# A three-layer kernel: up steps split around the first half of the down step, y's rest copied whole, and another order of roundings, splits and turnings

## The chip, the cores and the metric

The kernel runs on one core of a Trainium2 chip. The metric is device time in microseconds, the median of three runs. Five engines work side by side: PE (matrix products, with PEld for its weight loads), DVE and ACT (elementwise work out of both memories), POOL (elementwise work in SBUF) and SP (which issues all DMAs here).

## The reference

A causal convolution of 7 taps per head (softmax weights) is followed by two dense blocks, each with an up product to 2048 columns, a gate, and a down product back to 192.

```python
w = softmax(weight, axis=-1)                          # [8 heads, 7 taps]
x = conv(x_pad, w)                                    # [8192 tokens, 192]
h = x @ moe_w_in                                      # up 1, to 2048
g = where(h >= 1, h, where(h <= -1, 0, (h + 1)**2 / 4))
y = g @ moe_w_out                                     # down 1, back to 192
h = y @ moe2_w_in                                     # up 2
out = (h * sigmoid(1.702 * h)) @ moe2_w_out           # down 2
```

Everything is fp32. The kernel splits each factor of a product into a rounded part (hi) and its residue (lo) and adds three products of these.

## The kernel before, in words

**Tiles and steps.** The 8192 tokens are 16 tiles of 512. A step is one tile and one of 16 column blocks of 128 (F_TILES); `Step.n` counts steps from 0 to 255. Block 1 works on step n while block 2 works on step n - 24 (BEHIND). The time between two steps is called a slot here, and s is its number within a tile. Slots 0 to 23 are solo slots with block 1 alone. From slot 24 on, slots are paired. Tiles 0 to 3 are written out (`run_head`), tiles 4 to 13 are a loop of pairs, the rest is `run_tail`.

**A paired slot on PE.** Each product is cut into two halves of 64 rows of the array. One block works in the lower half while the other works in the upper half, then they change sides, which is called the flip here. A slot issues `end_up` of the step before (10 products, from L743), `begin_up` (8, from L717), then `down_both` for the step two slots back (LAG): a first half of 10 (L775 to L801), the flip, and a second half of 10 (L805 to L817). That is 38 products of half height, or 19 pairs. Behind a flip, PE waits for its own earlier products into the same bank: L805 waits `main_half` (set by L791), L807 `main2_half` (L793), L813 `rest_half` (L800), L815 `rest2_half` (L801), L743 `h1_half` (L731).

**What feeds it.** In each slot ACT runs two gelu passes of block 2 (L998, L1001), the square (L984) and the rounding of the gate (L990, g_hi). DVE runs the residue of the gate of the step before (L1153, g_lo), the clip (L1138), block 2's residue (L1159) and the gate (L1147). The first down product with g_lo is L791.

**The border of a tile.** When tile t's last down step has ended, ACT copies y's main part (L1008) and the upper half of the rest (L1010, into `y_part`); DVE takes the main residue (L1169), adds the lower half of the rest out of PSUM (L1173) and later takes the rest's residue (L1177); ACT rounds the rest (L1013). The next tile's down step starts in the same banks: L775 waits for L1169, L796 for L1173. That is slot s = 2.

**x of the next tiles.** POOL convolves (`convolve`, L532 and L539), SP moves blocks through DMAs (`move_x`), DVE turns them (`turn_x`, L1197), ACT rounds (`round_x`, L1035) and DVE splits (`split_x`, L1203, L1206), in slots named by the tables EARLY (tiles from 3), MIDDLE (tile 2) and LATE (tile 1).

**The start.** x of tile 0 is turned on PE out of two loads, the main part and the halo (`x_halo`), and convolved on DVE, ACT and POOL. Weights come in 16 chunks: ACT rounds chunk n (`split_weights`, L1044, in the slots of SPLIT_SLOTS), then POOL takes its residue (L564, L565, L568, L587), or DVE for chunk 0 (L1222). POOL also convolves tile 1, helped by ACT (SECOND_SLOTS); PE turns that tile in slot FIRST_PREP_STEP = 15 (`transpose_x`, L910), and step 16 needs it.

## Time and profile before

| what | value |
|---|---|
| runs (3) | 1156.56 us median, 1155.65 to 1156.84 |
| profiled execution | 1157.11 us, span 1155.4 us |
| PE busy | 1138.2 us (99%) |
| DVE, ACT, POOL busy | 822.9 (71%), 699.5 (61%), 446.7 (39%) us |
| mean granted TensorE clock | 0.999 |
| solo slots 0 to 23 | about 16 to 82 us |
| paired slots 24 to 255 | 82 to 1086 us |
| tail, block 2 alone | 1086 to 1155 us |

Matmuls are pipelined, so a product's length (0.39 us) is not its cost; the distance between starts is. The profile's busy share of PE therefore says little, and the time has to be read from distances between starts in the timeline.

### The profile page before, as it was taken

The page shows a single profiled execution, that of the slowest core. Times are in us where ns is not written, and L with a number is a line of the kernel's source. Part 1 is how long each engine was busy: PE and PEld are TensorE (multiplying, and loading weights), DVE is VectorE, ACT ScalarE, POOL GpSimd, SP SyncE. Part 2 cuts the span into 40 slices and gives each one's busy share as a digit, 9 for nine tenths or more (in the row PEclk, how much of TensorE's full clock was granted, in tenths as well). Part 3 has the DMA queues.
Part 4 walks back from the last instruction along what each step waited for, and adds up shares of the span by engine and source line. Part 5 has one row for each costly group of instructions (what it writes and reads, how often), then busy time and mean ns, then how long its engine had stood idle before and what let it go on. Part 6 is the DMA issues. An engine that isn't in the chain of part 4 may idle for free.

```text
span 1155.4 us, 25586 instructions
## 1 busy us (share of the span) xinstructions
PE 1138.2 (99%) x9384; PEld 1024.1 (89%) x9384; DVE 822.9 (71%) x1191; ACT 699.5 (61%) x1213; POOL 446.7 (39%) x441
## 2 busy tenths in 40 slices
PE   7999999999999999999999999999999999999998
PEld 4767899999989999899999999989999999989987
DVE  6877777777777777776777777777777777766633
ACT  5876566566666566565566666565665565655554
POOL 5997654170723608054170622608044180000000
PEclk9999999999999999999999999999999999999999
DMA  6312102020020200102020020200202010000000
GB/s 196 99 37 76 42 12 57 3 53 12 11 53 1 57 7 15 49 4 58 3 51 13 10 54 2 56 8 15 49 3 58 3 17 14 10 6 1 15 7 23
DMA packets 108790, 36.43 MB, mean 32 GB/s; under 512 B 101012, under 2 KB 105490, under 8 KB 108688
## 3 DMA queue, kind: packets, MB, share of 16 engines
q1 hardware_dynamic: 108688, 34.93, 12.7%
q8 instruction: 81, 1.33, 0.5%
q14 instruction: 21, 0.17, 0.0%
HBM read 23.09 MB, written 6.29 MB: 25 GB/s over the span
## 4 chain that ended last, share of the span: by engine, by line
PE 89%; POOL 4%; DVE 2%; SPq 1%; ACT 1%; DMA 1%; issue 1%; DVEq 0%; POOLq 0%; ACTq 0%
PE acc_all L810 4%; PE acc_all L805 4%; PE acc_all L813 4%; PE h_all L743 4%; PE acc_all L808 4%; PE acc_all L816 4%; PE h_all L748 4%; PE h_all L750 4%; PE acc_all L793 4%; PE h_all L746 4%; PE h_all L752 4%; PE acc_all L787 4%; PE acc_all L789 4%; PE h_all L726 4%; PE h_all L728 4%; PE h_all L733 4%
## 5 line engine op out<-in xcount | busy, mean ns | idle before, releaser
L998 ACT ACTIVATE g_hi<-h_all 128x512 fp32r<-128x512 f32 x256 | 153.1, 598 | 203.1 <-PE h_all L754 177.5
L1159 DVE TENSOR_TENSOR g_lo<-h_all,g_hi 128x512 fp32r<-128x512 f32 x256 | 176.7, 690 | 121.2 <-ACT h_all L1001 120.2
L1153 DVE TENSOR_TENSOR g_lo<-gate,g_hi 128x512 fp32r<-128x512 f32 x232 | 184.4, 795 | 110.2 <-ACT g_hi L990 104.3
L990 ACT ACTIVATE g_hi<-gate 128x512 fp32r<-128x512 f32 x232 | 146.5, 631 | 169.3 <-DVE gate L1147 166.0
L1138 DVE TENSOR_SCALAR clip<-h_all 128x512 f32<-128x512 f32 x256 | 175.9, 687 | 51.4 <-PE h_all L752 47.3
L532 POOL TENSOR_TENSOR x_conv<-x_in,tap_w 128x384 f32<-128x384 f32 (+1 forms) x29 | 30.1, 1058 | 458.2 <-DVE x_rest_a L1206 238.0
L539 POOL TENSOR_TENSOR x_conv<-x_conv,prod 128x384 f32<-128x384 f32 (+1 forms) x174 | 203.8, 1192 | 1.6
L984 ACT ACTIVATE clip<-clip,half 128x512 f32<-128x512 f32 x256 | 183.0, 715 | 17.6 <-DVE clip L1138 16.7
L1147 DVE TENSOR_TENSOR gate<-h_all,clip 128x512 f32<-128x512 f32 x232 | 160.4, 691 | 13.2 <-ACT clip L984 7.3
L1001 ACT ACTIVATE h_all<-h_all 128x512 f32<-128x512 f32 x256 | 151.8, 593 | 0.0
L532 POOL TENSOR_TENSOR prod<-x_in,tap_w 128x384 f32<-128x384 f32 (+1 forms) x174 | 149.8, 884 | 3.2
L546 POOL TENSOR_TENSOR raw<-raw,y_part 64x512 f32<-64x512 f32 x15 | 19.3, 1287 | 189.9 <-ACT y_part L1024 189.9
L807 PE MATMUL acc_all<-g_hi,w_down 64*128 64x512 f32 x231 | 91.0, 394 | 0.0
L799 PE MATMUL acc_all<-g_hi,w_down 64*128 64x512 f32 x231 | 90.7, 393 | 0.0
L805 PE MATMUL acc_all<-g_hi,w_down 64*128 64x512 f32 x231 | 90.6, 392 | 0.0
L796 PE MATMUL acc_all<-g_hi,w_down 64*128 64x512 f32 x231 | 90.4, 392 | 0.1
L800 PE MATMUL acc_all<-g_lo,w_down 64*128 64x512 f32 x231 | 90.5, 392 | 0.0
L811 PE MATMUL acc_all<-g_lo,w_down 64*128 64x512 f32 x231 | 90.5, 392 | 0.0
L791 PE MATMUL acc_all<-g_lo,w_down 64*128 64x512 f32 x231 | 89.8, 389 | 0.7 <-DVE g_lo L1153 0.4
L813 PE MATMUL acc_all<-g_hi,w_down 64*128 64x512 f32 x231 | 90.1, 390 | 0.0
L815 PE MATMUL acc_all<-g_hi,w_down 64*128 64x512 f32 x231 | 90.1, 390 | 0.0
L808 PE MATMUL acc_all<-g_hi,w_down 64*128 64x512 f32 x231 | 90.0, 390 | 0.0
(282 smaller groups left out, 4757.6 us busy)
## 6 DMA issues: line engine op xcount, KB each, us to landing
x_in<-in_x SPq DMA_DIRECT2D x14, 960.0 KB, 4.8
out_y<-raw SPq DMA_DIRECT2D x360, 16.0 KB, 1.4
raw<-x_conv SPq DMA_DIRECT2D x336, 16.0 KB, 1.8
raw<-in_moe_w_out SPq DMA_DIRECT2D x6, 384.0 KB, 3.6
raw<-in_moe_w_in SPq DMA_DIRECT2D x4, 512.0 KB, 4.4
raw<-in_moe_w_in SPq DMA_DIRECT2D x8, 256.0 KB, 4.6
stage<-in_moe_w_out SPq DMA_DIRECT2D x2, 384.0 KB, 6.9
x_in<-in_x SPq DMA_DIRECT2D x1, 768.0 KB, 9.0
```

Source lines behind the costliest of these rows:

```text
L532: ins = nc.gpsimd.tensor_tensor(by_head(dst, j), by_head(x_in, k + j), w, ALU.mult)
L539: ins = nc.gpsimd.tensor_tensor(o, o, prod[k % 2][:, j:j + slabs, 0:width], ALU.add)
L805: nc.tensor.matmul(main1, w1_main[UPPER, :], hi1[UPPER, :], start=False, stop=False)
L813: nc.tensor.matmul(rest1, w1_rest[UPPER, :], hi1[UPPER, :], start=False, stop=False)
L984: nc.scalar.activation(c, c, ACT.Square, bias=half[:, :], scale=0.5).then_inc(square_ready, 1)
L990: nc.scalar.activation(g1_hi[step.s % G_RING][:, :], gate1_of(step)[:, :], ACT.Copy).then_inc(g1_hi_ready, 1)
L998: nc.scalar.activation(g2_hi[step.s % G_RING][:, :], src, ACT.Gelu_apprx_sigmoid).then_inc(g2_hi_ready, 1)
L1001: nc.scalar.activation(src, src, ACT.Gelu_apprx_sigmoid).then_inc(gate2_ready, 1)
L1138: nc.vector.tensor_scalar(clip[step.s % 2][:, :], bank1(step)[:, :], -1.0, 1.0, ALU.max, ALU.min).then_inc(clip_ready, 1)
L1147: nc.vector.tensor_tensor(gate1_of(step)[:, :], bank1(step)[:, :], clip[step.s % 2][:, :], ALU.max).then_inc(gate1_ready, 1)
L1153: nc.vector.tensor_tensor(g1_lo[k][:, :], gate1_of(step)[:, :], g1_hi[k][:, :].bitcast(FP32), ALU.subtract).then_inc(g1_lo_ready, 1)
L1159: nc.vector.tensor_tensor(g2_lo[k][:, :], bank2(step)[:, :], g2_hi[k][:, :].bitcast(FP32), ALU.subtract).then_inc(g2_lo_ready, 1)
```

## The change

1. **PE.** `begin_up` keeps its first four products; the other four become `go_on_up`. `down_both` is cut at the flip into `begin_down` and `end_down`. In slots from 48 on (CALM_FROM) the order is `begin_up`, `begin_down`, `go_on_up`, `end_down`, but where either down step is the first of its tile (s = 2 and s = 10), and before slot 48, it stays as it was.
2. **y's rest.** From tile 1 on, ACT copies all 128 rows of the rest to `y_part` and later shifts its upper half into `y_shift` (`shift_y_rest`); POOL adds the halves (`sum_y`, from tile 2 on; DVE for tile 1). PE waits for ACT's copy (`y_from_act`), no longer for DVE's sum.
3. **x of the next tile.** `round_x` stands ahead of the slot's gate rounding, no longer behind it. EARLY turns in slots 5 and 6 (4 and 5 before); LATE spreads turns, roundings and splits over slots 13 to 15.
4. **Start.** The weights' first loads wait for the halo. ACT rounds chunks 1 and 3 ahead of the first slot, and chunk 4 in slots 0 and 1; the later chunks of block 1 move a slot up, chunks 14 and 15 a slot down. DVE takes chunk 0's residue in another order. FIRST_PREP_STEP is 14. POOL's share of chunk 15 goes into tile 3's convolution. Three warm-up products of 256 columns are added in `first_up`.

```diff
-    FIRST_PREP_STEP = 15
+    FIRST_PREP_STEP = 14
...
+        y_shift = raw[1][0:DR, TT:2 * TT]
...
+        CALM_FROM = 3 * F_TILES
...
-        EARLY = dict(turn={4: [0], 5: [1]}, hi={5: [0], 6: [1]}, lo={7: [0], 8: [1]})
+        EARLY = dict(turn={5: [0], 6: [1]}, hi={5: [0], 6: [1]}, lo={7: [0], 8: [1]})
...
-        LATE = dict(turn={13: [0, 1]}, hi={13: [0, 1]}, lo={14: [0, 1]})
+        LATE = dict(turn={13: [0]}, turn_in_slot={14: [1]}, hi={13: [0], 14: [1]}, lo={14: [0], 15: [1]})
...
+            sp.wait_ge(x_halo, 16 * BATCH)
             for n in range(5):
                 load_raw(n)
...
+            def sum_y(tile):
+                pool.wait_ge(y_shifted, tile)
+                y_rest = y_part[0:DR, :]
+                nc.gpsimd.tensor_tensor(y_rest, y_rest, y_shift, ALU.add).then_inc(y_summed, 1)
+                pool.wait_ge(y_summed, tile + 1)
...
             def prepare(tile):
+                if sums_on_pool(tile - 1):
+                    sum_y(tile - 1)
...
+                for _ in range(3):
+                    warm_up(TT // 2)
                 pe.wait_ge(x_from_dve, 2)
...
                 if first1:
-                    pe.wait_ge(y_from_dve, one.tile * 3 - 1)
+                    pe.wait_ge(y_from_act, one.tile * 3 - 1)
...
-                if n is None or n >= BEHIND + LAG:
-                    down_both(back(tile, side, s, LAG), back(tile, side, s, BEHIND + LAG))
+                later = down1_.s == 0 or down2_.s == 0 or n is not None and n < CALM_FROM
+                if later:
+                    go_on_up(up1_, up2_)
+                begin_down(down1_, down2_)
+                if not later:
+                    go_on_up(up1_, up2_)
+                end_down(down1_, down2_)
...
+                elif part == 1 and copies_y(tile):
+                    nc.scalar.activation(y_part[:, :], rest_acc[:, :], ACT.Copy).then_inc(y_from_act, 1)
...
+            def shift_y_rest(tile):
+                act.wait_ge(y_from_act, tile * 3 + 2)
+                nc.scalar.activation(y_shift, y_part[DR:P, :], ACT.Copy).then_inc(y_shifted, 1)
...
-            SPLIT_SLOTS = {0: [(3, None)], 1: [(4, 0)], 2: [(4, 1)], 5: [(5, 0), (5, 1)], 7: [(6, 0), (6, 1)],
-                           9: [(7, 0), (7, 1)], 14: [(8, 0)], 16: [(8, 1)], 18: [(9, 0)], 19: [(9, 1)],
+            SPLIT_SLOTS = {0: [(4, 0)], 1: [(4, 1)], 4: [(5, 0), (5, 1)], 6: [(6, 0), (6, 1)],
+                           8: [(7, 0), (7, 1)], 14: [(8, 0)], 16: [(8, 1)], 18: [(9, 0)], 19: [(9, 1)],
...
-                if takes_y(tile) and not solo and s == 1:
-                    take_y(tile - 1, 1 - side, 1)
```

**PE, an ordinary slot from 48 on, around the flip.** In these rows x and y are the moving operands of the up products, g_hi and g_lo those of the down products. Before:

```order
L791 MATMUL acc_all<-g_lo,w_down 128x512 [waits g1_lo_ready]
L793 MATMUL acc_all<-g_lo,w_down 128x512 [waits g2_lo_ready]
L796 MATMUL acc_all<-g_hi,w_down 128x512
L799 MATMUL acc_all<-g_hi,w_down 128x512
L800 MATMUL acc_all<-g_lo,w_down 128x512
L801 MATMUL acc_all<-g_lo,w_down 128x512
L805 MATMUL acc_all<-g_hi,w_down 128x512 [waits main_half]
L807 MATMUL acc_all<-g_hi,w_down 128x512 [waits main2_half]
```

The same place after the change:

```order
L825 MATMUL acc_all<-g_lo,w_down 128x512 [waits g1_lo_ready]
L827 MATMUL acc_all<-g_lo,w_down 128x512 [waits g2_lo_ready]
L830 MATMUL acc_all<-g_hi,w_down 128x512
L833 MATMUL acc_all<-g_hi,w_down 128x512
L834 MATMUL acc_all<-g_lo,w_down 128x512
L835 MATMUL acc_all<-g_lo,w_down 128x512
L763 MATMUL h_all<-x_hi_b,in_lo 128x512
L764 MATMUL h_all<-y_hi_a,in_lo 128x512
L765 MATMUL h_all<-x_rest_b,rest_hi 128x512
L767 MATMUL h_all<-y_rest_a,rest_hi 128x512
L848 MATMUL acc_all<-g_hi,w_down 128x512 [waits main_half]
L850 MATMUL acc_all<-g_hi,w_down 128x512 [waits main2_half]
```

Four up products now stand between the first half of the down step and the waits for its own products; the first half, with its waits for g_lo, comes four products sooner.

**ACT, the border of a tile in the loop.** Before (L1010 is the copy of half the rest, L984 and L990 with gate_1 belong to the next slot):

```order
L1008 ACTIVATE y_hi_a<-acc_all 128x512 [waits down1_done]
L989 REGISTER_ALU [waits gate1_ready]
L990 ACTIVATE g_hi<-gate_0 128x512 [waits down1_done]
L1010 ACTIVATE y_part<-acc_all 64x512
L995 REGISTER_ALU
L998 ACTIVATE g_hi<-h_all 128x512 [waits down2_done,h2_ready]
L1001 ACTIVATE h_all<-h_all 128x512
L982 REGISTER_ALU
L984 ACTIVATE clip<-clip,half 128x512 [waits clip_ready]
L990 ACTIVATE g_hi<-gate_1 128x512 [waits down1_done,gate1_ready]
```

After:

```order
L1060 ACTIVATE y_hi_a<-acc_all 128x512 [waits down1_done]
L1041 REGISTER_ALU [waits gate1_ready]
L1042 ACTIVATE g_hi<-gate_0 128x512 [waits down1_done]
L1062 ACTIVATE y_part<-acc_all 128x512
L1047 REGISTER_ALU
L1050 ACTIVATE g_hi<-h_all 128x512 [waits down2_done,h2_ready]
L1053 ACTIVATE h_all<-h_all 128x512
L1034 REGISTER_ALU
L1036 ACTIVATE clip<-clip,half 128x512 [waits clip_ready]
L1070 ISA
L1071 ACTIVATE raw<-y_part 64x512 [waits y_from_act]
L1042 ACTIVATE g_hi<-gate_1 128x512 [waits down1_done,gate1_ready]
```

The copy has all 128 rows, and the shift (L1071, `raw` is `y_shift`) stands ahead of the next slot's gate rounding; DVE's L1173 has no counterpart there.

**ACT, the last rows ahead of the first slots and these.** Before (L1044 rounds weights; the square L984 marks a slot):

```order
L1044 ACTIVATE rest_hi<-raw 128x256 [waits raw_loaded1]
L1121 ACTIVATE x_rest_a<-y_part 64x512 [waits upper_in_place,lower_in_place]
L1044 ACTIVATE rest_hi<-raw 128x768 [waits raw_loaded1]
L1044 ACTIVATE w_down<-stage 128x4x192 [waits staged0]
L984 ACTIVATE clip<-clip,half 128x512 [waits clip_ready]
L1044 ACTIVATE w_down<-stage 128x4x192 [waits staged1]
L990 ACTIVATE g_hi<-h_all 128x512 [waits gate1_ready]
L984 ACTIVATE clip<-clip,half 128x512 [waits clip_ready]
L1044 ACTIVATE in_hi<-raw 128x512 [waits raw_loaded2]
L990 ACTIVATE g_hi<-h_all 128x512 [waits gate1_ready]
L984 ACTIVATE clip<-clip,half 128x512 [waits clip_ready]
L1044 ACTIVATE in_hi<-raw 128x512 [waits raw_loaded2]
```

After:

```order
L1102 ACTIVATE rest_hi<-raw 128x256 [waits raw_loaded1]
L1102 ACTIVATE rest_hi<-raw 128x768 [waits raw_loaded1]
L1181 ACTIVATE x_rest_a<-y_part 64x512 [waits upper_in_place,lower_in_place]
L1102 ACTIVATE w_down<-stage 128x4x192 [waits staged0]
L1102 ACTIVATE w_down<-stage 128x4x192 [waits staged1]
L1036 ACTIVATE clip<-clip,half 128x512 [waits clip_ready]
L1102 ACTIVATE in_hi<-raw 128x512 [waits raw_loaded2]
L1042 ACTIVATE g_hi<-h_all 128x512 [waits gate1_ready]
L1036 ACTIVATE clip<-clip,half 128x512 [waits clip_ready]
L1102 ACTIVATE in_hi<-raw 128x512 [waits raw_loaded2]
```

Both halves of chunk 4 (`in_hi` from `raw_loaded2`) stand one slot sooner, and chunks 1 and 3 stand ahead of all slots.

## Rows read from the trace of the kernel before

**Rows 1.** The page: its head, and the chain that ended last, by engine.

```profile
span 1155.4 us, 25586 instructions
...
PE 89%; POOL 4%; DVE 2%; SPq 1%; ACT 1%; DMA 1%; issue 1%; DVEq 0%; POOLq 0%; ACTq 0%
```

**Rows 2.** Timeline of a paired slot: start us, length us, engine, line, operation.

```profile
599.73 0.39 PE L717 MATMUL h_all<-x_hi_a,in_hi 64*128 64x512 f32 x1
...
601.09 0.39 PE L791 MATMUL acc_all<-g_lo,w_down 64*128 64x512 f32 x1
...
601.53 0.18 PEld L805 LDWEIGHTS acc_all<-g_hi,w_down 64*128 64x128 f32 x1
...
602.93 0.39 PE L745 MATMUL h_all<-y_hi_b,in_hi 64*128 64x512 f32 x1
...
603.14 0.69 DVE L1153 TENSOR_TENSOR g_lo<-gate,g_hi 128x512 fp32r<-128x512 f32 x1 [0.70 <-ACT g_hi L990]
...
604.06 0.39 PE L717 MATMUL h_all<-x_hi_b,in_hi 64*128 64x512 f32 x1
```

**Rows 3.** Timeline of PE, first matmul of three slots 1 and 15 slots apart.

```profile
890.65 0.39 PE L717 MATMUL h_all<-x_hi_b,in_hi 64*128 64x512 f32 x1
...
895.10 0.39 PE L717 MATMUL h_all<-x_hi_b,in_hi 64*128 64x512 f32 x1
...
960.10 0.39 PE L717 MATMUL h_all<-x_hi_a,in_hi 64*128 64x512 f32 x1
```

**Rows 4.** Timeline at the border behind tile 8: ACT, DVE and PE.

```profile
612.91 0.60 ACT L1010 ACTIVATE y_part<-acc_all 64x512 f32<-64x512 f32 x1
...
613.61 0.68 DVE L1173 TENSOR_TENSOR y_part<-acc_all,y_part 64x512 f32<-64x512 f32 x1
...
614.34 0.49 PE L796 MATMUL acc_all<-g_hi,w_down 64*128 64x512 f32 x1
...
617.13 0.69 DVE L1153 TENSOR_TENSOR g_lo<-gate,g_hi 128x512 fp32r<-128x512 f32 x1 [0.70 <-ACT g_hi L990]
...
618.55 0.39 PE L791 MATMUL acc_all<-g_lo,w_down 64*128 64x512 f32 x1
```

**Rows 5.** Waits: engine, tile, line, awaited; us in total, times, longest.

```profile
PEld acc_all L796 <- DVE y_part L1173: 3.7, 14, 0.4
```

**Rows 6.** Timeline at 116 us: a DVE subtraction beside POOL's convolution.

```profile
116.74 2.13 POOL L532 TENSOR_TENSOR prod<-x_in,tap_w 128x384 f32<-128x384 f32 x2
...
116.84 1.30 DVE L1153 TENSOR_TENSOR g_lo<-gate,g_hi 128x512 fp32r<-128x512 f32 x1 [0.70 <-ACT g_hi L990]
```

**Rows 7.** Timeline of the passage into paired slots, 87 to 135 us.

```profile
87.48 0.50 PE L717 MATMUL h_all<-x_hi_b,in_hi 64*128 64x512 f32 x1 [0.16 <-DVE gate L1147]
...
101.12 0.94 ACT L1044 ACTIVATE w_down<-raw 128x384 fp32r<-128x384 f32 x2 [2.06 <-DMA raw<-in_moe_w_out]
...
113.59 1.24 DVE L1206 TENSOR_TENSOR x_rest_a<-raw,x_rest_a 64x512 fp32r<-64x512 f32 x1
...
116.29 0.47 PE L717 MATMUL h_all<-x_hi_a,in_hi 64*128 64x512 f32 x1 [0.70 <-DVE gate L1147]
...
135.16 0.39 PE L717 MATMUL h_all<-x_hi_a,in_hi 64*128 64x512 f32 x1
```

**Rows 8.** Timeline of the start, 9 to 60 us: PE, ACT and POOL.

```profile
9.43 0.66 PE L883 MATMUL acc_all<-ident,x_in 128*128 128x128 f32 x4 [1.86 <-DMA x_in<-in_x]
...
26.55 0.62 ACT L1044 ACTIVATE in_hi<-raw 128x512 fp32r<-128x512 f32 x1
...
27.24 2.41 POOL L568 TENSOR_TENSOR in_lo<-raw,in_hi 128x1024 fp32r<-128x1024 f32 x1 [1.82 <-ACT in_hi L1044]
...
56.36 0.30 PE L910 MATMUL acc_all<-ident,x_conv 128*128 128x128 f32 x1 [1.41 <-POOL x_conv L599]
...
59.57 0.50 PE L653 MATMUL h_all<-x_hi_b,in_hi 128*128 128x512 f32 x1 [0.97 <-DVE x_rest_b L1215]
```

**Rows 9.** Stretches: length, busy of PE PEld DVE ACT POOL, clock, DMA.

```profile
18.70:22.10 3.40, 3.19 (x8) 2.48 (x8) 3.37 (x4) 1.31 (x3) 3.10 (x3) 0.50 0.78 150
```

More of the change, by code:

```diff
@@ L283, in takes_y, with copies_y, sums_on_pool @@
             return not isinstance(tile, int) or 1 <= tile <= TILES
+        def copies_y(tile):
+            return not isinstance(tile, int) or tile >= 1
+        def sums_on_pool(tile):
+            return not isinstance(tile, int) or tile >= 2
         def takes_out(tile):
@@ L621, in _ @@
             convolve(2, slabs=2, between={2: [8], 3: [9], 4: [10]})
-            for n in range(11, 2 * N_CHUNKS):
+            for n in range(11, 2 * N_CHUNKS - 1):
                 split_weights(n)
@@ L698, in up2 @@
                 if step.s == 0:
-                    pe.wait_ge(y_from_dve, (step.tile + 1) * 3)
+                    pe.wait_ge(y_from_dve, (step.tile + 1) * 2)
                 pe.wait_ge(g2_lo_ready, step.n - 1)
@@ L720, in begin_up @@
                 if two.s == 0:
-                    pe.wait_ge(y_from_dve, (two.tile + 1) * 3)
+                    pe.wait_ge(y_from_dve, (two.tile + 1) * 2)
                 if isinstance(two.n, int) and two.n < 2:
@@ L1090, in slot @@
                     take_out(tile - 2, 0)
+                if takes_y(tile) and at_y == 1 and copies_y(tile - 1):
+                    shift_y_rest(tile - 1)
+                if prepares(tile):
+                    for part in prep(tile)["hi"].get(s, ()):
+                        round_x(tile + 1, 1 - side, part)
                 if one is not None:
@@ L1100, in slot @@
                     take_out(tile - 2, 2)
-                if prepares(tile):
-                    at = prep(tile)
-                    for part in at["hi"].get(s, ()):
-                        round_x(tile + 1, 1 - side, part)
             act.wait_ge(tap_step, 2)
@@ L1235, in slot @@
                 at_y = s - shift_y(tile)
-                if takes_y(tile) and not solo and at_y == 3:
+                if takes_y(tile) and not solo and at_y == 2 and not sums_on_pool(tile - 1):
+                    sum_y(tile - 1)
+                if takes_y(tile) and not solo and at_y == 4:
                     take_y(tile - 1, 1 - side, 2)
@@ L1242, in slot @@
                     turn_rest(tile - 2)
-                if prepares(tile) and not is_late(tile):
+                if prepares(tile):
                     prepare_x(tile, side, s)
@@ L1259, in slot @@
                 if is_late(tile):
-                    prepare_x(tile, side, s)
+                    for part in LATE["turn_in_slot"].get(s, ()):
+                        turn_x(tile + 1, part)
                 if two is not None:
```

66 lines of the change are left out of this document (46 added, 20 removed), and 2 rows, old and new, of the table SPLIT_SLOTS.

## The prediction

> **What bounds the kernel now.** I read the page's head and chain first, then the timeline of PE, then the waits, then the start. The chain that ended last lies 89% on PE [rows 1], so an edit is worth what it takes out of PE's distances between starts, and an elementwise operation counts only where PE waits for its result. The profiled execution took 1157.11 us, 0.55 above the median of 1156.56; sums below are made against it and carried to the median.
>
> An ordinary paired slot lasts (960.10 - 895.10)/15 = 4.333 us [rows 3]. From L717 to L791 are six pairs of products in 1.36 us, 0.2267 a pair; from L745 to the next L717 five pairs take 1.13, the same [rows 2]. Nineteen pairs would make 4.307. So 0.0267 us are lost in each slot, and they lie between L791 and L745, where eight pairs take 1.84 us and not 1.813 [rows 2]. In that stretch is the flip with its wait of L805 for L791's end. L791 ends at 601.48 and the weights of L805 load at 601.53 [rows 2]: the wait is a real one. The other change of halves, between the up steps, waits for nothing that was just issued, and it lies in the five pairs that show no loss.
>
> A border slot (s = 2) lasts 895.10 - 890.65 = 4.45 [rows 3], 0.12 above an ordinary one. There L796 waits for DVE's sum L1173, 3.7 us in 14 times [rows 5]. Two more places lose time: the passage into paired slots, where ten slots take 135.16 - 87.48 = 47.68 us [rows 7], 4.35 above ten ordinary ones, and the start, where PE waits for x of tile 1 in two steps [rows 8].
>
> **PE's order.** No product is added in paired slots; four move. After the change two more pairs, 0.45 us, stand between the first half's products and the waits for them at the flip. That is over ten times the loss, so I let the loss go whole. It holds for slots 48 to 255 without s = 2 and s = 10 of thirteen tiles: 208 - 26 = 182 slots, 182 x 0.0267 = **-4.85 us** (bounds 0, if the loss isn't the wait, and -4.85). The price: L791 reads g_lo 0.45 us sooner. Before, L1153 ended at 603.83 in the slot shown [rows 2], and the next L791 comes at 601.09 + 4.333 = 605.42, a lead of 1.59; 1.14 remain. The slots at s = 2 and s = 10, whose leads are shorter, keep the order of before. Slot s = 3 is weighed below.
>
> **The border.** L796 now waits for ACT's copy. L1010 ended at 612.91 + 0.60 = 613.51 [rows 4]; a copy of all 128 rows has the same 512 elements a row, and ACT's operations of 128x512 take about the same (0.62 in [rows 8]), so it ends 0.8 us before L796's start, at 614.34. DVE's sum ended at 613.61 + 0.68 = 614.29, 0.05 before that product. The wait goes, and the next one, for g_lo, is that of L791 in the same slot, which is ahead of L796. 13 x 0.12 = 1.5 is the whole excess of such slots; some borders show less of it (the mean wait of [rows 5] is 0.26 against a longest of 0.4), so I take **-1.2** (bounds 0 and -1.5).
>
> Behind the border, L791 at s = 3 starts at 618.55 and its g_lo (L1153) ended at 617.13 + 0.69 = 617.82 [rows 4]: a lead of 0.73. It is read 0.45 + 0.12 sooner now. ACT's shift, some 0.60, stands ahead of the rounding that L1153 waits for; queued behind it are that rounding, x's or y's next rounding and block 2's gelu passes, and DVE's subtraction waits for the first. Against that, DVE loses L1173 (0.68), which stood ahead of the clip, so clip, square and gate come up to 0.6 us sooner; the shift then fits into ACT's wait for the gate. POOL's addition follows the shift and may run beside L1153: beside POOL it took 1.30 and not 0.69 [rows 6], 0.61 longer. So the lead is 0.73 - 0.57 + about 0.45 - 0.61 = about 0.0, where PE just doesn't wait. I take **0** (bounds 0 and +5, which is 13 x 0.4).
>
> In rows 6 the subtraction starts 0.10 behind the first of two POOL operations of 2.13/2 = 1.07 us and is 0.61 longer than alone, less than the 0.97 that were left of that one. The Trainium skill ("SBUF — State Buffer", section "SBUF: two separate sides") calls the port pair that VectorE and GpSimd share an exclusive lock, held for the whole instruction of whoever comes first. That speaks against the sum on POOL: by it the hold could be as long as the addition, and it is one of the rivals below.
>
> Two more edits with one answer: `round_x` goes into ACT's wait for the gate, and EARLY's turns move a slot down into DVE's 0.70 wait for g_hi [rows 2]. Both are hidden there, at 0; where that cover is gone, each would hold g_lo by its own length, 0.6 to 0.7 us, against a lead of 1.14.
>
> **The passage into paired slots.** PE's order is as before up to slot 48. Chunk 14 is rounded a slot later, so ACT's wait of 2.06 for its load [rows 7] goes; PE stood behind it only in part, and I put 0.6 of the 4.35 to it, an estimate between 0 and 2.06. The two splits of x of tile 2, among them L1206 (1.24 beside POOL), stood in one slot, and L717 waited 0.70 behind them [rows 7]; spread over two slots that wait goes, -0.7. The border of tile 1 may give some 0.3 more, as two or three of the 0.12 above. Sum **-1.6** (bounds 0 and -2.5). Most of the 4.35 stays: POOL's convolutions still run beside DVE there [rows 6].
>
> **The start.** POOL waits 1.82 us for ACT's second half of chunk 4, at 26.55 + 0.62 = 27.17, before L568 [rows 8]. That half now comes one solo slot sooner (10 products x 0.227 = 2.27, of which I count 2.1), and so does POOL's chain to x of tile 1, which PE met with waits of 1.41 at L910 and 0.97 at L653 [rows 8]. The transposes also move to slot 14: PE waits there longer (2 to 3 us, as an estimate from 56.36 less 2.1 and a slot of products that are no longer ahead of it), but the wait before step 16 has 15 products (3.4 us) instead of 5 in front of it and goes. Step 16, at 59.57 before, comes at about 58.5: **-1.05**. Bounds: -2.1, the whole lead of the chain; and above nothing, since PE ran at half clock for 3.4 us at 18.7 [rows 9], behind waits at the start. A clock that falls in the same way during the longer wait costs 3.4/2 = 1.7. The weights' loads now wait for the halo; PE waits for x until 9.43 anyway, 1.86 of it on DMA [rows 8], so loads behind it are late by at most that, and with less beside it x may land sooner by as much: 0, from -1.86 to +1.86. I take the row's middle, since the loads' own uses come ten us later. The three warm-up products stand in a wait of PE, at 0.
>
> **Sum.** -4.85 - 1.2 - 1.6 - 1.05 + 0 = -8.70. The profiled execution would be 1148.4, the median 1156.56 - 8.70 = 1147.9, which is the predicted time (0.75% less).
>
> **Rivals.** *The flip's loss isn't the wait.* If changing sides in the same bank costs 0.0267 us by itself, the first term is 0 and the time 1152.7. For it: only this flip writes the banks of the products just issued. Against it: the load of L805 follows 0.05 behind the end of L791 [rows 2], as a wait would make it. 13%.
>
> *The start gives nothing, or the clock falls.* +1.7 instead of -1.05: 1147.9 + 2.75 = 1150.7. For it: rows 9, and a longer wait than before in slot 14. Against it: PE has run for 30 us by then, and the waits of 1.41 and 0.97 [rows 8] had no such fall behind them. 14%.
>
> *Both fail.* The split around the down step then doesn't do what it says, and the start costs: 1147.9 + 4.85 + 2.75 = 1155.5, the same as before. 8%.
>
> *POOL's addition holds DVE's subtraction for its whole length.* At 1.07 and not 0.61, each border is 0.46 late, and 13 x 0.46 = 6.0 us: 1153.9. For it: both would start within some tenths of a microsecond. Against it: the 0.61 of rows 6. The page of the Trainium skill named above would make it so. 4%.
>
> *Slower: g_lo is late behind each border.* If DVE comes no sooner, the shift (0.60) and POOL's hold (0.61) fall on L1153 alone: 0.73 - 0.57 - 0.60 - 0.61 = -1.05, and thirteen borders cost 13.7 us: 1147.9 + 13.7 = 1161.6. It decides from 8.70/13 = 0.67 us of lateness per border. Against it: L1173 did stand on DVE ahead of that slot's clip [rows 4]. 6%.
>
> **How the numbers follow.** The forecast has 55%, with a range of its own from 1145.6 (the start at -2.1, the passage at -2.5) to 1150.5 (a border at +2.6). About 0.2%, 2.3 us, is what a measurement can tell from no change here. Faster by more, below 1154.2: 55 + 13 + 14 + 4 = 86%. Same: 8%. Slower, above 1158.9: 6%. The range of 8 in 10 takes in the forecast and the first two rivals, 1145.5 to 1153.0, and leaves out the others, 4 + 8 + 6 = 18%.
>
> **What would show it.** In the trace of after, ordinary slots should be 4.307 apart, with nine pairs between the first half and the flip evenly spaced and the loss gone; still 4.333 there would prove the first rival. Slots at s = 2 should come down from 4.45 to 4.333, with no wait at L830 for y. L825 at s = 3 should start without a wait for g_lo; idle time of half a microsecond there would be the slower rival. Slots 29 and 31, in the passage, should be near 4.4. Step 16 should start near 58.5, with the granted clock at 1.0 behind the transposes. I would be wrong above all if shorter leads of g_lo turn up as new small waits in many slots.

## The result, and the profile of the changed kernel

The changed kernel takes 1148.94 us (median of six runs, 1148.06 to 1150.79) where the kernel before takes 1156.47 in the same comparison: 0.9941 of it, interval 0.9928 to 0.9954. A second comparison on another chip (e12 below) gave 1148.43, 0.9929 [0.9916, 0.9943]. The forecast was 1147.9. The profiled execution took 1148.50, so 8.61 less than the profiled one before, where the sum said 8.70.

The page's head and the chain by engine, to be read against [rows 1]:

```profile
span 1146.8 us, 25607 instructions
...
PE 92%; POOL 3%; DVE 2%; DMA 1%; ACT 1%; issue 0%; SPq 0%; DVEq 0%; POOLq 0%; ACTq 0%
```

The time splits at the starts of PE's slots, read from the first up product of each (L717 before, L745 after):

| stretch | before, us | after, us | difference | forecast |
|---|---|---|---|---|
| start, to slot 24 | 82.18 | 81.24 | -0.94 | -1.05 |
| slots 24 to 47 | 105.00 | 103.63 | -1.37 | -1.6 |
| slots 48 to 254 | 898.83 | 892.17 | -6.66 | -6.05 |
| slot 255 to PE's end | 65.48 | 65.44 | -0.04 | 0 |
| behind PE's end | 3.88 | 4.29 | +0.41 | 0 |

An ordinary slot on PE, start, length, line (answers [rows 2]; L825 is the first down product with g_lo, L848 the first behind the flip, L777 the first of `end_up`):

```profile
615.89 0.39 PE L745 MATMUL h_all<-x_hi_b,in_hi 64*128 64x512 f32 x1
...
616.80 0.39 PE L825 MATMUL acc_all<-g_lo,w_down 64*128 64x512 f32 x1
...
617.81 0.39 PE L848 MATMUL acc_all<-g_hi,w_down 64*128 64x512 f32 x1
...
618.94 0.39 PE L777 MATMUL h_all<-x_hi_b,in_hi 64*128 64x512 f32 x1
...
620.20 0.39 PE L745 MATMUL h_all<-x_hi_b,in_hi 64*128 64x512 f32 x1
```

The slot takes 4.31, read finer 4.3067 (4.306 or 4.307 in each such slot from 48 on): nineteen pairs and nothing else. Slots s = 2 and s = 10, which kept the old order, take 4.333 each. One of them, s = 2 of tile 9, for the 4.45 of [rows 3]:

```profile
607.25 0.39 PE L745 MATMUL h_all<-x_hi_b,in_hi 64*128 64x512 f32 x1
611.58 0.39 PE L745 MATMUL h_all<-x_hi_b,in_hi 64*128 64x512 f32 x1
```

The border behind tile 8, by ACT, POOL, DVE and PE (answers [rows 4]):

```profile
607.18 0.59 ACT L1062 ACTIVATE y_part<-acc_all 128x512 f32<-128x512 f32 x1
609.47 0.63 ACT L1071 ACTIVATE raw<-y_part 64x512 f32<-64x512 f32 x1
```

```profile
610.18 1.29 POOL L561 TENSOR_TENSOR y_part<-y_part,raw 64x512 f32<-64x512 f32 x1 [13.04 <-ACT raw L1071]
```

```profile
610.94 1.08 DVE L1213 TENSOR_TENSOR g_lo<-gate,g_hi 128x512 fp32r<-128x512 f32 x1 [0.70 <-ACT g_hi L1042]
```

```profile
608.61 0.39 PE L825 MATMUL acc_all<-g_lo,w_down 64*128 64x512 f32 x1
608.84 0.39 PE L830 MATMUL acc_all<-g_hi,w_down 64*128 64x512 f32 x1
...
612.49 0.39 PE L825 MATMUL acc_all<-g_lo,w_down 64*128 64x512 f32 x1
```

ACT's copy ends at 607.77, 1.07 ahead of L830, so the wait of [rows 5] is gone. DVE's subtraction behind the border is held by POOL's addition (1.08 for 0.69). It ends at 612.02, and L825 at s = 3 reads it at 612.49: a lead of 0.47, where the prediction had 0.0. At the thirteen borders the lead is 0.41 to 0.47.

The passage into paired slots (answers [rows 7]; the starts of slots 26, 31, 32 and 36):

```profile
86.57 0.50 PE L745 MATMUL h_all<-x_hi_b,in_hi 64*128 64x512 f32 x1 [0.18 <-DVE gate L1207]
...
109.13 0.39 PE L745 MATMUL h_all<-x_hi_b,in_hi 64*128 64x512 f32 x1
114.87 0.49 PE L745 MATMUL h_all<-x_hi_a,in_hi 64*128 64x512 f32 x1 [0.79 <-DVE x_rest_a L1271]
...
132.88 0.39 PE L745 MATMUL h_all<-x_hi_a,in_hi 64*128 64x512 f32 x1
```

The ten slots take 46.31 for 47.68. But slot 31 takes 114.87 - 109.13 = 5.74; before it was 5.39. That is this execution: in e12, the same kernel, it takes 5.09, and slot 44 takes 4.87 where it is 4.33 here. Among all profiles in which POOL's convolution for tile 3 wasn't moved, slot 31 takes 5.05 to 5.74.

The start, PE's waits (answers [rows 8]), then DVE and POOL behind x's rest:

```profile
8.91 0.65 PE L926 MATMUL acc_all<-ident,x_in 128*128 128x128 f32 x4 [1.27 <-DMA x_in<-in_x]
...
20.47 0.50 PE L700 MATMUL h_all<-x_rest_a,rest_hi 128*128 128x512 f32 x1 [1.73 <-DVE x_rest_a L1382]
...
54.44 0.30 PE L953 MATMUL acc_all<-ident,x_conv 128*128 128x128 f32 x1 [2.04 <-POOL x_conv L619]
...
58.78 0.39 PE L676 MATMUL h_all<-x_hi_b,in_hi 128*128 128x512 f32 x1
```

```profile
18.65 1.77 DVE L1382 TENSOR_TENSOR x_rest_a<-y_part,x_rest_a 64x512 fp32r<-64x512 f32 x1 [1.31 <-ACT x_rest_a L1181]
```

```profile
17.37 2.49 POOL L607 TENSOR_TENSOR rest_lo<-raw,rest_hi 128x256 fp32r<-128x256 f32 x2 [0.77 <-ACT rest_hi L1102]
...
25.37 2.40 POOL L588 TENSOR_TENSOR in_lo<-raw,in_hi 128x1024 fp32r<-128x1024 f32 x1 [0.99 <-ACT in_hi L1102]
```

Step 16 starts at 58.78, 0.79 sooner than before. POOL reaches chunk 4 1.87 sooner (25.37 for 27.24), but PE's first step ends later: step 1 starts at 21.04, 0.98 later than before. The halo's products come 0.52 sooner here (8.91 for 9.43) with the weights held back; e6 below weighs that.

### The profile page after: what moved, and what is told of

The parts are those of the page before. It is cut to its first block, busy times and chain, and to the rows that moved or that the text cites. A ratio compares the mean times of both kernels' runs of the same rounds, so it can differ in the third digit from the quotient of the medians.

```text
span 1146.8 us, 25607 instructions
## 1 busy us (share of the span) xinstructions
PE 1130.0 (99%) x9390; PEld 1091.1 (95%) x9390; DVE 816.5 (71%) x1177; ACT 705.6 (62%) x1228; POOL 464.8 (41%) x455
## 3 DMA queue, kind: packets, MB, share of 16 engines
q8 instruction: 81, 1.33, 0.5%
## 4 chain that ended last, share of the span: by engine, by line
PE 92%; POOL 3%; DVE 2%; DMA 1%; ACT 1%; issue 0%; SPq 0%; DVEq 0%; POOLq 0%; ACTq 0%
PE h_all L782 2%; PE h_all L780 2%; PE h_all L777 2%; PE acc_all L856 2%; PE h_all L786 2%; PE acc_all L853 2%; PE acc_all L851 2%; PE h_all L784 2%; PE acc_all L848 2%; PE acc_all L859 2%; PE acc_all L835 2%; PE acc_all L833 2%; PE acc_all L821 2%; PE acc_all L827 2%; PE acc_all L823 2%; PE h_all L754 2%
## 5 line engine op out<-in xcount | busy, mean ns | idle before, releaser
L1213 DVE TENSOR_TENSOR g_lo<-gate,g_hi 128x512 fp32r<-128x512 f32 x232 | 184.1, 794 | 105.2 <-ACT g_hi L1042 99.1
L561 POOL TENSOR_TENSOR y_part<-y_part,raw 64x512 f32<-64x512 f32 x14 | 18.0, 1284 | 217.0 <-ACT raw L1071 217.0
L825 PE MATMUL acc_all<-g_lo,w_down 64*128 64x512 f32 x231 | 89.6, 388 | 0.6 <-DVE g_lo L1213 0.4
L827 PE MATMUL acc_all<-g_lo,w_down 64*128 64x512 f32 x231 | 89.6, 388 | 0.0
L852 PE MATMUL acc_all<-g_hi,w_down 64*128 64x512 f32 x231 | 89.5, 388 | 0.0
L858 PE MATMUL acc_all<-g_hi,w_down 64*128 64x512 f32 x231 | 89.4, 387 | 0.0
L848 PE MATMUL acc_all<-g_hi,w_down 64*128 64x512 f32 x231 | 89.4, 387 | 0.0
L850 PE MATMUL acc_all<-g_hi,w_down 64*128 64x512 f32 x231 | 89.4, 387 | 0.0
L860 PE MATMUL acc_all<-g_lo,w_down 64*128 64x512 f32 x231 | 89.4, 387 | 0.0
L856 PE MATMUL acc_all<-g_hi,w_down 64*128 64x512 f32 x231 | 89.3, 387 | 0.0
L853 PE MATMUL acc_all<-g_lo,w_down 64*128 64x512 f32 x231 | 89.3, 386 | 0.0
L834 PE MATMUL acc_all<-g_lo,w_down 64*128 64x512 f32 x231 | 89.3, 386 | 0.0
```

Source lines behind the costliest of these rows:

```text
L827: nc.tensor.matmul(main2, w2_main[UPPER, :], lo2[UPPER, :], start=False, stop=False).then_inc(main2_half, 1)
L848: nc.tensor.matmul(main1, w1_main[UPPER, :], hi1[UPPER, :], start=False, stop=False)
L1213: nc.vector.tensor_tensor(g1_lo[k][:, :], gate1_of(step)[:, :], g1_hi[k][:, :].bitcast(FP32), ALU.subtract).then_inc(g1_lo_ready, 1)
```

## The experiments

My theory is the sum of the prediction: the wait at the flip, the wait for DVE's sum at the border, and the start. Its rivals were that the loss at the flip belongs to the change of sides, that POOL's addition or the shift gives the border's gain back, and that the clock falls in the longer wait ahead of the turning. All kernels are the changed one with the edit shown. Line numbers shift by a few from kernel to kernel.

**e1: the split undone.**

```diff
-                later = down1_.s == 0 or down2_.s == 0 or n is not None and n < CALM_FROM
+                later = True
```

> The changed kernel with the four up products ahead of the down step in every slot, as before the change; all else stays. If the loss at the flip is the wait for the half's own products, ordinary slots go from 4.307 back to 4.333 us, 182 of them, and the four slots at the loop's back edge, which also became shorter in the changed kernel, get some 0.1 each back: 4.85 + 0.5, so about 1153.9 against 1148.5 in the profiled execution. If the gain came from the border, from DVE or from the leads of g_lo, ordinary slots stay at 4.307 and the time at 1148.5.

Measured: 1154.2 us (1153.67 to 1155.47), 0.9972 [0.9963, 0.9982] of the kernel before on its chip. The profiled execution took 1155.04. An ordinary slot on PE:

```profile
554.67 0.39 PE L745 MATMUL h_all<-x_hi_a,in_hi 64*128 64x512 f32 x1
559.01 0.39 PE L745 MATMUL h_all<-x_hi_a,in_hi 64*128 64x512 f32 x1
```

Slots are at 4.333 again, and so are those at s = 2, without the border's 0.12. The slots at the loop's back edge are longer again by 0.06 to 0.14. From slot 48 to 255 it takes 897.41, 5.24 more than the changed kernel (5.35 expected). The rest of the 6.5 stands at the start: step 16 came at 60.10 here and not at 58.78, though nothing was changed there. The windows of 54 to 58 us (columns as in [rows 9]) of the changed kernel and of this one:

```profile
54.00:58.00 4.00, 3.56 (x20) 3.13 (x21) 2.16 (x4) 2.19 (x4) 2.71 (x4) 1.00 0.05 19
```

```profile
54.00:58.00 4.00, 3.86 (x15) 3.31 (x16) 1.68 (x3) 1.45 (x4) 2.33 (x3) 0.58 0.01 4
```

The granted clock was 0.58 behind the wait of 2.06 us at L953: near the lower level for most of the stretch. That is the second rival of the prediction, in one execution and not in the other.

**e2: other distances to the wait.** Go_on_up's two pairs are issued ahead of the down step's first half (first) or behind it (second), and the main products with g_lo can stand last in that half:

```diff
+                if later or loop and side == 0 or not loop and tile == TILES - 1:
+                    first, second = (0, 1), ()
+                elif loop:
+                    first, second = (0,), (1,)
+                else:
+                    first, second = (), (0, 1)
...
+                main_last = not later and not loop and tile >= TILES - 2
```

> The changed kernel with another distance between the first half's main products and the wait for them in different tiles, counted in pairs of products. Loop tiles of side 0: no split, 3 pairs. Loop tiles of side 1: only one pair of up products moved, 4 pairs. Tile 3: as changed, 5 pairs. Tile 14: split, but the main products with g_lo put last in the half, 3 pairs. Tile 15: no split and these products last, 1 pair. If it is the wait, the slot follows the distance alone: 4.333 at 3 pairs, 4.307 at 4 pairs (the loss of 0.027 is far below a pair of 0.227), 4.307 at 5, 4.333 in tile 14 too, and 0.027 + 2 x 0.227 = 0.48 more, 4.79, in tile 15. If it is the change of sides itself, which products of another bank between the halves soften, 4 pairs give half of it, 4.320, tile 14 stays at 4.307 and tile 15 at 4.333.

Measured, in ordinary slots: 4.333 at 3 pairs (side 0), 4.307 at 4 pairs (side 1), 4.307 at 5 (tile 3), 4.333 in tile 14, and 4.707 in tile 15, with one pair. A slot of side 1 (tile 7), one of tile 14 and one of tile 15:

```profile
372.58 0.39 PE L745 MATMUL h_all<-x_hi_b,in_hi 64*128 64x512 f32 x1
376.89 0.39 PE L745 MATMUL h_all<-x_hi_b,in_hi 64*128 64x512 f32 x1
...
968.98 0.39 PE L745 MATMUL h_all<-x_hi_a,in_hi 64*128 64x512 f32 x1
973.32 0.39 PE L745 MATMUL h_all<-x_hi_a,in_hi 64*128 64x512 f32 x1
...
1035.10 0.39 PE L745 MATMUL h_all<-x_hi_b,in_hi 64*128 64x512 f32 x1
1039.81 0.39 PE L745 MATMUL h_all<-x_hi_b,in_hi 64*128 64x512 f32 x1
```

The slot follows the distance alone, also where the up products stand between the halves (tile 14). The change of sides costs nothing. Only the size at one pair was off: 0.40 above the least and not 0.48. (The one run took 1158.94. Of the 10.4 above the changed kernel's profile, 5.2 are tile 15's longer slots and 2.2 the slots at 3 pairs; another 2.3 stand ahead of slot 24, where the granted clock fell twice.)

**e3: the border as before.**

```diff
         def copies_y(tile):
-            return not isinstance(tile, int) or tile >= 1
+            return False
...
-                    pe.wait_ge(y_from_act, one.tile * 3 - 1)
+                    pe.wait_ge(y_summed, one.tile)
...
+                if takes_y(tile) and not solo and s == 1:
+                    take_y(tile - 1, 1 - side, 1)
```

> The changed kernel with the border of a tile as before: ACT copies half of y's rest, DVE adds the other half out of PSUM ahead of its clip, PE waits for that sum, and neither ACT's shift nor POOL's addition is there. If the sum on DVE was what the product L830 waited for, slots at s = 2 go from 4.333 to about 4.45, 13 x 0.10 to 0.12: 1.3 to 1.5 more, 1149.9 for 1148.5. Ordinary slots stay at 4.307. If the new way of the rest costs as much elsewhere (POOL's hold of DVE, the shift on ACT), the time doesn't change or falls.

Measured: 1150.91 us (1150.66 to 1151.64), 0.9945 [0.9929, 0.9962]. The profiled execution took 1150.74. The slot at s = 2 of tile 8 and the wait as in [rows 5] (L826 is the product, L1229 DVE's sum):

```profile
539.77 0.39 PE L741 MATMUL h_all<-x_hi_a,in_hi 64*128 64x512 f32 x1
544.23 0.39 PE L741 MATMUL h_all<-x_hi_a,in_hi 64*128 64x512 f32 x1
```

```profile
PEld acc_all L826 <- DVE y_part L1229: 4.1, 14, 0.4
```

These slots take 4.45 to 4.47 again; ordinary ones stay at 4.307. Slots 48 to 254 take 1.78 more than in the changed kernel (1.3 to 1.5 expected). In tile 2 two slots are longer too, 34 (5.25) and 42 (4.98). So the new way of y's rest gives PE at least what I took for it. Behind PE's end this run takes 3.88 again, for 4.29.

**e4: the start as before** (the start's part of the diff above, reversed).

> The changed kernel with the start as before: loads of weights that don't wait for the halo, chunks 1 and 3 and the halves of chunk 4 in the old slots, tile 1 turned in slot 15, DVE's old order for chunk 0, no warm-up products in the first step. The first paired slot starts at 82.18 us in the kernel before and at 81.24 in the changed one, so 0.94 more: 1149.4 for 1148.5, if nothing of it is absorbed by a later wait. If the passage behind it absorbs it, the same as the changed kernel.

Measured: 1149.83 us (1149.67 to 1150.21), 0.9935 [0.9919, 0.9952]. The profiled execution took 1149.67, and slot 24 starts at 82.25, as before the change. In time this isn't to be told from the changed kernel (0.9929 and 0.9941). Its four runs lie within 0.54 us, those of the changed kernel within 2.7 and 3.6. So in the median no gain of the new start is shown. In the profiles with the new start, whole or without one of its pieces (e5, e6, e7), and the turning in slot 14, slot 24 starts at 80.67 to 81.46 where the clock didn't fall behind the wait for x of tile 1, and at 82.56 to 84.24 where it did, which is later than with the old start.

**e5: no warm-up products in the first step.**

```diff
-                for _ in range(3):
-                    warm_up(TT // 2)
```

> The changed kernel without the three warm-up products in its first step. If they hold the clock, PE runs at half clock for some us around 20 to 24 us, as the kernel with the old start did (granted 0.64 there), and step 7 starts 1.3 to 1.7 later than 34.9 to 35.2. At step 16 most of it is gone, since PE waits 2.04 us for x of tile 1 anyway; what stays is the part by which ACT rounds chunk 4 later in slots 0 and 1: step 16 at 59.0 to 59.5 for 58.5 to 58.8, so 0.5 to 0.8 more in all. If they do nothing, step 7 at 35 and no difference.

Measured: 1150.27 us (1149.55 to 1151.64), 0.9946 [0.9931, 0.9961]. The windows at 20 and at 54 us:

```profile
20.00:24.00 4.00, 3.98 (x9) 3.10 (x10) 2.70 (x4) 1.76 (x4) 3.90 (x4) 0.50 0.85 195
54.00:58.00 4.00, 3.41 (x15) 2.91 (x16) 2.10 (x4) 2.41 (x5) 2.71 (x4) 0.75 0.13 56
```

Without them PE runs at the lower level around 22 us. With them it is 1.00 there in nine of eleven profiles, and 0.75 and 0.68 in the other two (e2, e12). The three profiles without them (the kernel before, e4, e5) all have a fall there. So they go with a rarer fall and don't exclude it. Step 7 starts at 35.53, only 0.3 to 0.6 later. POOL's chain was 0.15 later (L953 at 54.59), less than the profiles with an unaltered start differ by (53.89 to 56.02). The loss was covered by the wait at L953, as expected, and the fall behind that wait hides what is left.

**e6: loads of weights that don't wait for the halo** (the line with `x_halo` of the diff above taken out).

> The changed kernel in which the loads of weights don't wait for the halo. The halo's transposes (L925) start at 9.4 again and not at 8.9, 0.5 later, as in the kernel before; ACT's wait of 1.52 us for chunk 1 goes. If the halo's landing sets the first step, steps 1 and 16 come 0.5 later: 0.5 more in all. If chunk 1's landing does, by way of x's rest, step 1 comes up to 1 us sooner than 21.0, POOL's chain too, and the time falls by 0.5. In my sum it was 0, between the two.

Measured: 1149.52 us (1148.77 to 1150.45), 0.9937 [0.9922, 0.9952], the same as the changed kernel. The halo's products start at 9.58, 0.67 later, step 1 at 21.27 (0.23 later) and the turning at 54.67 (0.23 later). But the profiles with the hold in place have the halo's products anywhere from 8.71 to 9.51, and those with the unaltered start have step 1 at 20.45 to 22.49 and the turning at 53.89 to 56.02. So the time agrees with the 0 of the sum; whether two effects cancel or neither is there, one profile can't tell. Step 16 came at 60.63 here, behind a fall of the clock (0.61 in 54 to 58 us).

**e7: x's rest rounded between the pieces of chunk 1.**

```diff
             split_weights(1, 0)
-            split_weights(1, 1)
             act.wait_ge(lower_in_place, 1)
             act.wait_ge(upper_in_place, 1)
             nc.scalar.activation(x_rest[DR:P, :], x_rest_sum, ACT.Copy).then_inc(x_from_act, 1)
+            split_weights(1, 1)
```

> The changed kernel with one line moved: ACT rounds x's rest between the two pieces of chunk 1, as before the change, not behind both. In the changed kernel DVE's residue of x's rest (L1382) ran beside POOL's second residue of chunk 1 and took 1.77 us, ending 0.56 behind POOL's end, and PE waited 1.73 for it. If that meeting is the cause, the residue takes 0.69 here, PE's wait shrinks to some 0.3 and step 1 starts 1.2 to 1.5 sooner; ACT's slots 0 and 1 and POOL's chunk 4 follow 0.5 to 1.0 sooner, and step 16 comes at 57.7 to 58.2 for 58.5 to 58.8: 0.6 less in all. If POOL's own work sets its chain, step 16 stays, PE waits 3.5 us and not 2.04 for x of tile 1, and the clock may fall more often.

Measured: 1150.76 us (1150.3 to 1151.67), 0.9952 [0.9937, 0.9968]. DVE, POOL and PE:

```profile
18.82 0.69 DVE L1382 TENSOR_TENSOR x_rest_a<-y_part,x_rest_a 64x512 fp32r<-64x512 f32 x1 [0.69 <-ACT x_rest_a L1180]
```

```profile
19.73 1.86 POOL L607 TENSOR_TENSOR rest_lo<-raw,rest_hi 128x768 fp32r<-128x768 f32 x1 [1.89 <-ACT rest_hi L1102]
```

```profile
55.18 0.30 PE L953 MATMUL acc_all<-ident,x_conv 128*128 128x128 f32 x1 [3.44 <-POOL x_conv L619]
```

The meeting is gone (0.69 for 1.77), and step 1 starts at 20.13, 0.9 sooner. But POOL now waits 1.89 for ACT's second piece, and its chain comes 0.74 later at L953, later than in any profile whose clock hadn't fallen by then. PE waits 3.44 there, the clock falls to 0.80 in 54 to 58 us, and step 16 starts at 61.10. My theory of this run was wrong: POOL's chain sets step 16, and what PE gains ahead of it is lost in the wait.

**e8: tile 1 turned in slot 15.**

```diff
-    FIRST_PREP_STEP = 14
+    FIRST_PREP_STEP = 15
```

> The changed kernel with tile 1 turned in slot 15, as before the change; the rest of the new start stays. In two of four profiles of kernels with the new start the clock fell to half behind PE's wait of 2.06 us ahead of the turning (0.58 in 54 to 58 us), and step 16 started at 60.1 and 61.1; in the other two at 58.5 and 58.8. A slot later PE comes at about 55.5, when x of tile 1 is there: the wait goes, the clock doesn't fall, and step 16 starts at 58.6 to 58.9 each time. So the median is that of the changed kernel's undisturbed executions, 1148.1 to 1148.6 on a chip on which the kernel before takes 1156.5 (ratio 0.993), and its runs lie closer together. If the turning a slot sooner is worth what I took for it, 1.05, the time rises by that instead.

Measured: 1148.45 us, all five runs from 1147.88 to 1149.08, 0.9929 [0.9916, 0.9943]. Step 16 and the window:

```profile
58.12 0.50 PE L676 MATMUL h_all<-x_hi_b,in_hi 128*128 128x512 f32 x1 [1.54 <-DVE x_rest_b L1280]
```

```profile
54.00:58.00 4.00, 2.58 (x16) 1.81 (x14) 3.69 (x6) 3.27 (x6) 2.70 (x5) 1.00 0.05 19
```

The wait ahead of the turning is gone, and PE waits 1.54 ahead of step 16 instead. Step 16 starts at 58.12, no later than in any profile with the turning in slot 14 (58.23 to 59.01 where the clock didn't fall). So turning tile 1 a slot sooner isn't what gained at the start. The rest of the new start is, since with the old one (e4) step 16 came at 59.52; that it is POOL's chain and none of the other moves is a reading of the waits and wasn't run by itself.

**e9: y's halves added by DVE.** `sums_on_pool` returns False, and POOL's three sums of the tail go.

> The changed kernel with the halves of y's rest added by DVE in every tile, out of SBUF, ahead of its subtraction at s = 2, and no addition on POOL. In the changed kernel that subtraction (L1213) takes 1.08 us at each border beside POOL's addition, and L825 at s = 3 reads g_lo with a lead of 0.44 us. If POOL's addition is what holds it, the subtraction takes 0.69 here; DVE's addition (0.69) fits into its wait of 0.70 for g_hi, and the lead is 0.7 to 0.8. PE waits in neither case, so slots from 48 on stay at 4.307 and 4.333 and the time stays the same. If DVE's addition isn't hidden, the lead falls under 0.2 and slots at s = 3 grow.

Measured: 1150.2 us (1148.7 to 1152.84), 0.9944 [0.9927, 0.996]. DVE behind the border of tile 8 (L1242 is the addition):

```profile
609.07 0.67 DVE L1242 TENSOR_TENSOR y_part<-y_part,raw 64x512 f32<-64x512 f32 x1
609.85 0.69 DVE L1212 TENSOR_TENSOR g_lo<-gate,g_hi 128x512 fp32r<-128x512 f32 x1
```

The subtraction takes 0.69 and not 1.08, and the lead at s = 3 is 0.78. Slots from 48 on stay as they are but for two: 239 and 240 take 5.50 and 4.82, 1.7 us more together. DVE stood still ahead of the gate of that step, for nothing that the profile shows:

```profile
1011.58 0.69 DVE L1206 TENSOR_TENSOR gate<-h_all,clip 128x512 f32<-128x512 f32 x1 [2.65 <-issue]
```

Whether that belongs to the edit isn't shown. At the borders POOL's hold is real and costs PE nothing.

**e10: POOL's convolution for tile 3 behind the splits of x of tile 2.**

```diff
+            pool.wait_ge(x_from_dve, 6)
             convolve(3, slabs=2, between={1: [15]})
```

> The changed kernel in which POOL starts the convolution for tile 3 only when DVE has split x of tile 2. In the passage of the changed kernel DVE's subtractions beside that convolution take 1.35 to 1.37 us (L1268, L1213, L1271), slot 31 takes 5.74 us and slot 34 4.87. If POOL's hold of DVE is what PE waits for there, slot 31 falls to 4.4 to 4.7, and the ten slots 26 to 36 from 46.31 to about 45.3: 1.0 less, as long as x of tile 3 is still in time (else a new wait in slots 40 to 47 gives it back). If the splits of x themselves are late for another reason (ACT, DMA), slot 31 stays above 5.

Measured: 1149.42 us (1149.26 to 1153.94), 0.9942 [0.9919, 0.9964]. DVE and POOL in slots 30 to 41:

```profile
108.41 0.69 DVE L1269 TENSOR_TENSOR x_lo_a<-raw,x_hi_a 128x512 fp32r<-128x512 f32 x1 [0.58 <-ACT x_hi_a L1094]
...
112.40 0.69 DVE L1272 TENSOR_TENSOR x_rest_a<-raw,x_rest_a 64x512 fp32r<-64x512 f32 x1
...
155.37 0.71 DVE L1263 STREAM_TRANSPOSE raw<-raw 128x512 f32<-128x512 f32 x1 [4.19 <-DMA raw<-x_conv]
```

```profile
113.25 2.10 POOL L546 TENSOR_TENSOR x_conv<-x_in,tap_w 128x384 f32<-128x384 f32 x2 [7.23 <-DVE x_rest_a L1272]
```

Slot 31 takes 4.333, slot 34 4.37: the passage's loss behind slot 28 was DVE beside POOL. But x of tile 3 comes 6 us later. DVE waits 4.19 for its blocks at slot 40, g_lo is late, and slot 41 takes 6.99. The gain of 2 us is given back.

**e11 and e12: what the runs pointed to, put together, beside the changed kernel.** e11 has e8's and e10's edits, x of tile 3 turned in slots 42 and 43, the split from slot 28 on, and one pair moved at s = 2 and s = 10.

> The changed kernel with what the runs before point to: tile 1 turned in slot 15; POOL's convolution for tile 3 behind DVE's splits of x of tile 2, and x of tile 3 turned in slots 42 and 43 (40 and 42 in the changed kernel), so that DVE no longer waits for its blocks; the four up products behind the first half of the down step from slot 28 on, and one pair of them also at s = 2 and s = 10 from slot 48 on. Expected: slots 28 to 47 at 4.307 to 4.36 (slot 34, at the border, may stay above), with no slot of 7 us, so slots 24 to 48 in 101.2 for 103.63 us; slots at s = 2 and s = 10 at 4.307, 26 x 0.027 = 0.7 less; no fall of the clock behind the turning. In all 3.1 less than the changed kernel's profiled 1148.5, about 1145.4, a ratio of 0.990 to the kernel before. If the leads of g_lo at the border are too short for one pair (0.44 and 0.46 before, 0.22 left), slots at s = 2 or s = 10 stay at 4.33 or grow; if POOL's later convolution meets DVE further on, slots 36 to 49 grow by up to 0.5 each.

> The changed kernel once more, unaltered, beside the combined one on the same chip. Expected: 0.9935 to 0.9945 of the kernel before, with runs up to 2.5 us apart, the longer ones at a lower mean granted clock (0.996 to 0.998), since the clock falls behind the turning of tile 1 in some executions and not in others.

Measured: e11 1150.89 us (1149.41 to 1152.1), 0.9949 [0.9935, 0.9963]; e12 1148.43 (1147.97 to 1151.55), 0.9929 [0.9916, 0.9943]. e11 was expected at 1145.4 and isn't faster than e12. Its slots 28 to 44 are at 4.306 to 4.42, but slot 45 takes 9.49. DVE and POOL ahead of it:

```profile
170.38 0.70 DVE L1261 STREAM_TRANSPOSE raw<-raw 64x512 f32<-64x512 f32 x1 [2.63 <-POOL raw L566]
```

```profile
169.07 1.28 POOL L566 TENSOR_TENSOR raw<-raw,y_part 64x512 f32<-64x512 f32 x1
```

POOL's next convolution starts later as well (161.71 for 155.11), and the sum of the output's halves (L566) stands inside it. DVE's turning of the output waits for that, and g_lo behind it. PE waits 3.29 for g_lo (L828 at 173.54), and behind that the clock fell, which is most of what the slot took beyond the wait:

```profile
174.00:178.00 4.00, 4.00 (x26) 3.13 (x24) 3.74 (x5) 1.98 (x3) 3.92 (x5) 0.57 0.12 18
```

One pair at s = 2 and s = 10 gave nothing: 4.31 to 4.40. The leads of g_lo there fell to 0.12 to 0.21, which the expectation named as the way to fail. None of these runs is faster than the changed kernel and e8. In e12's profile the clock fell again: L953 at 56.02 behind a wait of 2.40, 0.70 in the window, step 16 at 61.79. That profile is of e12's one long run (1151.55, mean granted clock 0.996; its other four took 1147.97 to 1148.88). The ratio came a little below the expected 0.9935 to 0.9945, and the runs lie 3.6 us apart where 2.5 was expected.

## Why the prediction was right, point by point

The profiled difference of 8.61 lies 0.09 from the sum, and that is closer than the terms are: by stretch they were off by -0.61 (from slot 48 on), +0.23 (the passage), +0.11 (the start), -0.04 (slot 255 to PE's end) and +0.41 (behind it), which nearly cancel. So the main mechanism is right, and the closeness is partly luck.

**The flip: right, and shown.** -4.85 was forecast for the loss, and ordinary slots went from 4.333 to 4.307; e2 shows that the distance to the wait does it and excludes the first rival. What the step left out are the loop's back edges: four slots were longer by 0.07 to 0.15 before and are not after, another -0.48. They come back with e1.

**The border: right, the size a little low.** -1.2 was forecast; the slots at s = 2 lost all of their 1.33, and e3 gives 1.78 with what follows in the next slots. The lead of g_lo at s = 3 was taken as 0.0 and is 0.47, since the subtraction is held for 0.39 and not 0.61 and ACT's rounding comes sooner. The slower rival falls with that. The rival on POOL's hold had the mechanism and not the price: DVE is held to the end of POOL's addition, but that starts 0.76 ahead of the subtraction, so 0.39 is left to pay, out of the lead. On its kind the Trainium skill ("SBUF — State Buffer", section "SBUF: two separate sides") is borne out: it says that a VectorE operation with two inputs in SBUF and a GpSimd operation that reads SBUF exclude each other for the whole instruction. L1213 ends 0.55 behind the end of POOL's addition (612.02 and 611.47), L1382 0.56 behind that of L607 (20.42 and 19.86), both started within it. The profiles of before and after have 152 meetings in which a subtraction of DVE out of SBUF starts within an operation of POOL with over 0.16 us of it left. In 151 it ends 0.54 to 0.56 behind POOL's; in one (at 128.51 in the changed kernel) it ran in 0.67, and POOL's operation took some 0.6 longer. The two subtractions with an input in PSUM (`acc_all`, L1277 and L1280 in the changed kernel) ran beside POOL in 0.69. How long DVE is held follows from when it starts, not from a price per meeting, and the 0.61 that I took from [rows 6] was one such case, which I read wrongly. Shown by itself, POOL's first operation there takes 0.86 and not 2.13/2 = 1.07:

```profile
116.74 0.86 POOL L532 TENSOR_TENSOR prod<-x_in,tap_w 128x384 f32<-128x384 f32 x1
```

It ends at 117.60, so 0.76 of it was left and not 0.97, and the subtraction ended behind it, at 118.14. [rows 6] spoke for a hold of the whole rest and not against it.

**The passage: the sum was near, one of its steps wrong.** -1.6 was forecast and -1.37 came. Slot 29 went from 5.11 to 4.33, 0.78 for the 0.6 of chunk 14 (no run moves that chunk alone); slots 32 and 34 gave 0.53 and 0.33, and slot 34 went back to 5.25 with the old border (e3). But spreading the two splits of x over two slots was to give 0.7 in slot 31, and that slot became 0.35 longer, or 0.30 shorter in e12. The splits still meet POOL (1.37 and 1.36), and the second now stands last ahead of the step that needs it; L745 waits 0.79 for it. e10 shows that without POOL beside it the slot takes 4.333.

**The start: the size near in this execution, the reasoning wrong.** Step 16 came 0.79 sooner, 1.05 was forecast. POOL's chain did come 1.9 sooner. But the turning in slot 14 doesn't bring it to PE: e8, with it in slot 15, reaches step 16 at 58.12. I counted 15 products behind the turning as a gain over 5, and left out that PE stands idle ahead of it in exchange. The second rival is real as a mechanism, and it isn't one case for all executions: the granted clock in 54 to 58 us was 1.00 in four profiles with the turning in slot 14 (the changed kernel, e3, e9, e10) and 0.58 to 0.80 in six (e1, e2, e5, e6, e7, e12), and 1.00 in all three with it in slot 15 (e4, e8, e11). Waits of 2.03 and 2.06 us stood ahead of both, so their length alone doesn't decide. Step 16 then starts at 60.10 to 61.79, and without the fall at 58.23 to 59.01. The changed kernel's longer runs (1150.54 and 1150.79) carry a mean granted clock of 0.996 and 0.997, its shorter ones 0.998 and 0.999. That fits, as e12's long run has a low clock and a profile that shows the fall, but no profile of those two runs is there. It accounts for about half of the 1.0 by which the median lies above the forecast: the other four runs have a median of 1148.4, 0.5 above.

**The end: a term that was missing.** Behind PE's last product 4.29 us follow for 3.88. All kernels with POOL's addition of y's halves have it and the three without don't, so the border's edit may pay it; why is open (below).
